# GpSimd's work on the weights tied to the steps of z, u's parts prepared a step earlier, and another order of the last pair

## What is computed

```python
theta = x @ w_theta
zr, zi = x * np.cos(theta), x * np.sin(theta)
y = einsum('ts,bsd->btd', w_tok_r, zr) + einsum('ts,bsd->btd', w_tok_i, zi)
u = x + y
u = u + np.maximum(u @ w_ch, 0.0)
h = np.maximum(u @ w_in, 0.0)
# conv over three neighbouring tokens, per channel, then
gate = 1.0 / (1.0 + np.exp(-conv_out))
out = (h * gate) @ w_out
```

## Time and profile before

| | us |
|---|---|
| median of 3 runs | 525.27 |
| lowest, highest | 524.72, 525.97 |
| the profiled execution, whole | 525.06 |
| its span, first to last instruction | 523.3 |
| TensorE busy (matmul) in the span | 507.9 |
| DVE, ACT, GpSimd busy | 441.4, 328.4, 89.7 |

### The profile page before, as it was taken

The page is one execution under the profiler, slowest core; times in us unless marked ns, Lnnn a source line. Parts: engine busy times, 40 slices in busy tenths (PEclk is TensorE's granted clock), DMA queues, the critical chain, the costliest instruction groups (busy, mean ns, idle before and its releaser), DMA issues.

```text
span 523.3 us, 10574 instructions
## 1 busy us (share of the span) xinstructions
PE 507.9 (97%) x4022; PEld 497.4 (95%) x4022; DVE 441.4 (84%) x682; ACT 328.4 (63%) x599; POOL 89.7 (17%) x76
## 2 busy tenths in 40 slices
PE   8999999999999998999799999999999999999997
PEld 7989898999999998999699999999999999999996
DVE  8999997999898869889588876898888888788783
ACT  4889887755534444354235364787777688678764
POOL 5988984000000142012000000000000000000000
PEclk9999999999999999999989999999999999999999
DMA  8999997999420732025600568002411002001102
GB/s 327 340 323 313 342 317 182 286 326 225 149 91 1 223 135 95 1 104 139 240 3 1 188 271 321 34 2 98 174 45 47 2 0 91 0 1 46 46 1 90
DMA packets 38114, 73.54 MB, mean 141 GB/s; under 512 B 6448, under 2 KB 23856, under 8 KB 38064
## 3 DMA queue, kind: packets, MB, share of 16 engines
q1 hardware_dynamic: 37344, 71.69, 41.2%
q10 hardware_dynamic: 720, 1.18, 0.6%
HBM read 52.80 MB, written 20.05 MB: 139 GB/s over the span
## 4 chain that ended last, share of the span: by engine, by line
PE 81%; DVE 9%; ACT 4%; DMA 3%; issue 2%; SPq 1%; POOL 0%; DVEq 0%; ACTq 0%
PE y_bank L1811 22%; PE y_bank L1897 17%; PE x_bank L1883 9%; PE theta_bank L1883 7%; PE y_bank L1842 7%; PE x_bank L1798 6%; PE weighed L1718 4%; PE x_sum L1676 4%; PE x_sum L1691 2%; DMA u_scratch<-u_part 2%; PE turned L1703 2%; DVE u_part L1502 1%; PE turned L1723 1%; PE x_sum L1662 1%; DVE angle L1432 1%
## 5 line engine op out<-in xcount | busy, mean ns | idle before, releaser
L1811 PE MATMUL y_bank<-rest_w,z 128*128 128x384 f32 x432 | 76.8, 335 | 1.5 <-DVE z L1460 1.5
L1811 PE MATMUL y_bank<-first_w,z 128*128 128x384 f32 x432 | 76.9, 334 | 0.3 <-issue 0.3
L1811 PEld LDWEIGHTS y_bank<-rest_w,z 128*128 128x128 f32 x432 | 74.9, 188 | 2.2 <-DVE z L1460 2.1
L1811 PEld LDWEIGHTS y_bank<-first_w,z 128*128 128x128 f32 x432 | 75.0, 188 | 0.5 <-issue 0.5
L1842 PE MATMUL y_bank<-u_part,channel_w 128*128 128x384 f32 x216 | 42.2, 345 | 4.2 <-DVE u_part L1502 4.2
L1137 ACT ACTIVATE sine<-angle 128x384 f32<-128x384 f32 x24 | 12.6, 526 | 52.3 <-DVE angle L1435 52.3
L1842 PEld LDWEIGHTS y_bank<-u_part,channel_w 128*128 128x128 f32 x216 | 39.1, 195 | 5.1 <-DVE u_part L1502 5.1
L1798 PE MATMUL x_bank<-theta_w,x_t 128*128 128x384 f32 x216 | 41.5, 335 | 0.2 <-DVE x_t L1417 0.2
L1798 PEld LDWEIGHTS x_bank<-theta_w,x_t 128*128 128x128 f32 x216 | 37.7, 188 | 0.7 <-DVE x_t L1417 0.7
L1718 PE MATMUL weighed<-q_scaled,k_scaled 64*128 64x128 f32 x384 | 31.6, 283 | 1.4 <-POOL q_scaled L986 1.0
L1718 PEld LDWEIGHTS weighed<-q_scaled,k_scaled 64*128 64x128 f32 x384 | 28.4, 187 | 4.1 <-issue 2.5
(11 more groups left out here) (213 smaller groups left out, 1215.9 us busy)
## 6 DMA issues: line engine op xcount, KB each, us to landing
u_scratch<-u_part SPq DMA_DIRECT2D x12, 768.0 KB, 4.3
first_w<-u_scratch SPq DMA_DIRECT2D x8, 768.0 KB, 7.7
a_in<-in_a_rows SPq DMA_DIRECT2D x15, 390.0 KB, 6.1
k_in<-in_k_rows SPq DMA_DIRECT2D x15, 384.0 KB, 6.0
q_in<-in_q_rows SPq DMA_DIRECT2D x14, 384.0 KB, 5.4
v_in<-in_v_tokens SPq DMA_DIRECT2D x16, 288.0 KB, 4.9
x_blocks<-x_scratch SPq DMA_DIRECT2D x12, 288.0 KB, 6.8
y<-x_even SPq DMA_DIRECT2D x6, 576.0 KB, 3.0
```

The lines of the kernel that those rows point to most:

```text
L1811: ins = pe.matmul(y_bank[2 * d + half][:, 0:HALF], z[s % 2][part][zp][:, d * P:(d + 1) * P], mixing_w(part, wp, s)[:, half_tokens(half)], ...
```

## The change

Three things are changed, all of them in order and waiting:

- **GpSimd's work on the weights** moves from `spare` to a `prepare_u` of its own, at spot 1 of steps 0 to 4, and starts in each with a wait for the split of z of the next tile, `z_low.done(pool, (b + 1) * T + s + 1)` (the b there is one less than the batch that is mixed). The two operations of double width are cut in two, so there are nine subtractions and four sums, 13 operations of 128 x 512. Tables `W_ROUNDED`, `W_SPLIT` and `W_COMBINED` say where each lies, by (batch mixed, step). The last two parts now belong to batch 3, and SP's load of w_out, which overwrites them, moves from step 0 to step 2 of batch 3, ahead of `load_u(0)`.
- **u's parts** are rounded, split, combined and stored from step 0 on: ACT's parts 0 and 1 stand at spot 0 of step 0 (before: spot 1 of step 0), the last at spot 0 of step 3 (before: step 4); DVE's splits and subtractions lie one or two spots to a step and a half earlier, the last at spot 1 of step 3; SP stores at spot 1 of steps 1 and 3 (before: 2 and 4). ACT waits for just as many subtractions as a part needs.
- **The last pair** of the feed-forward part: ACT rounds the odd tile's g ahead of the sigmoid of the even tile. DVE applies the odd tile's gate ahead of conv3 of the even tile, and splits the odd g ahead of the even tile's gate product.

```diff
@@ mix_batch @@
-            if b and not last:
+            if b:
                 do.spare(b, s)
@@ tables @@
-    N_W, N_U = 7, 5
+    N_W, N_U = 9, 5
-    W_OF = {(1, 2): (0,), (1, 3): (1,), (1, 4): (2,), (2, 2): (3, 4), (2, 3): (5, 6)}
+    W_PARTS = ("a12", "a22", "a11", "s1", "s3", "s2", "s4", "even", "odd")
+    W_ROUNDED = {(1, 1): (0, 1), (1, 3): (2,), (2, 1): (3,), (2, 2): (4, 5), (2, 3): (6,), (3, 0): (7, 8)}
+    W_SPLIT = {(1, 2): (0,), (1, 3): (1,), (1, 4): (2,), (2, 2): (3,), (2, 3): (4,), (2, 4): (5, 6), (3, 1): (7,), (3, 2): (8,)}
+    COMBINED = ("s1", "s3", "s2", "s4")
+    W_COMBINED = {(1, 4): (0,), (2, 0): (1,), (2, 1): (2,), (2, 2): (3,)}
@@ SP @@
-            if (s, spot) == (2, 1):
+            if (s, spot) == (1, 1):
                 u_split.done(sp, b, 3)
...
-            if (s, spot) == (4, 1):
+            if (s, spot) == (3, 1):
                 u_split.done(sp, b)
...
         def prepare(s):
-            if s == 0:
+            if s == 2:
                 sp.wait_ge(w_low, N_W)
                 sp.dma_start(out_rows[:, :, :], w_out.rearrange("(a p) n -> p a n", p=P)).then_inc(out_w_got, 16)
                 sp.dma_start(taps[:, :, :], taps_in).then_inc(taps_got, 16)
-            if s == 2:
                 mixed.done(sp, LAST * T + 1)
                 load_u(0)
@@ GpSimd @@
+        def split_w(m):
+            part = W_PARTS[m]
+            high, low = ff_w[part]
+            pool.wait_ge(w_high, m + 1)
+            pool.tensor_tensor(low, W_RAW[part], high.bitcast(F32), ALU.subtract).then_inc(w_low, 1)
+
+        def combine_w(i):
...
+            pool.wait_ge(w_low, 3)
+            if i:
+                pool.wait_ge(w_added, i)
+            pool.tensor_tensor(out, left, right, op).then_inc(w_added, 1)
+
+        def prepare_u(b, s, spot):
+            if spot == 1 and s < T - 1:
+                z_low.done(pool, (b + 1) * T + s + 1)
+                for m in W_SPLIT.get((b + 1, s), ()):
+                    split_w(m)
+                for i in W_COMBINED.get((b + 1, s), ()):
+                    combine_w(i)
@@ ACT @@
+            if m >= 3:
+                u_combined.done(act, b, 2 * m - 4)
             if m == 3:
-                u_combined.done(act, b)
...
-            for m in {(0, 1): (0, 1), (1, 1): (2,), (3, 1): (3,), (4, 0): (4,)}.get((s, spot), ()):
+            for m in {(0, 0): (0, 1), (0, 1): (2,), (2, 1): (3,), (3, 0): (4,)}.get((s, spot), ()):
                 round_u(b, m)
@@ ACT, step @@
+            if m == FF_STEPS - 1:
+                round_g(m, 1)
             if shapes:
                 gate(m, 0)
...
-            if shapes:
+            if m < FF_STEPS - 1:
                 round_g(m, 1)
@@ DVE @@
-            for m in {(1, 0): (0,), (1, 1): (1,), (2, 0): (2,), (4, 0): (3,), (4, 1): (4,)}.get((s, spot), ()):
+            for i in {(1, 1): (0, 1), (2, 0): (2,), (2, 1): (3,)}.get((s, spot), ()):
+                combine(b, i)
+            for m in {(0, 1): (0, 1), (1, 0): (2,), (3, 0): (3,), (3, 1): (4,)}.get((s, spot), ()):
                 split_part(b, m)
-            for i in {(2, 1): (0,), (3, 0): (1,), (3, 1): (2, 3)}.get((s, spot), ()):
-                combine(b, i)
@@ DVE, step @@
                 conv2(m, 0)
+            if m == FF_STEPS - 1:
+                apply_gate(m, 1)
+            if shapes:
                 conv3(m, 0)
+            if m == FF_STEPS - 1:
+                split_g(m, 1)
...
-            if shapes:
+            if m < FF_STEPS - 1:
                 apply_gate(m, 1)
...
             if shapes:
                 apply_gate(m, 0)
+            if m < FF_STEPS - 1:
                 split_g(m, 1)
```

More of the change, by code:

```diff
@@ L752, in layer @@
     U_COUNT = [16 * (4 + 1 + b % 2) for b in range(LAST)]
[L754 to L765 removed]
+    W_RAW = {"a12": w_raw[:, 1, :, 0, :], "a22": w_raw[:, 1, :, 1, :], "a11": w_raw[:, 0, :, 0, :], "s1": w_raw[:, 1, :, 1, :],
+             "s3": w_raw[:, 0, :, 1, :], "s2": w_raw[:, 0, :, 0, :], "s4": w_raw[:, 1, :, 0, :],
+             "even": w_raw[:, 2, :, 0, :], "odd": w_raw[:, 2, :, 1, :]}
+    W_PARTS = ("a12", "a22", "a11", "s1", "s3", "s2", "s4", "even", "odd")
[3 more added lines that the diff above has]
+    W_COMBINED = {(1, 4): (0,), (2, 0): (1,), (2, 1): (2,), (2, 2): (3,)}
     block = ctx.enter_context(nc.Block())
@@ L1013, in select @@
                                pattern=[[0, len(BLOCKS_OF) - EARLY], [1, CHUNK]], channel_multiplier=-1).then_inc(selected.sem, 1)
-        def spare(b, s):
-            for m in W_OF.get((b, s), ()):
-                pool.wait_ge(w_high, m + 1)
-                raw, (high, low) = w_part_of(m)
-                pool.tensor_tensor(low, raw, high.bitcast(F32), ALU.subtract).then_inc(w_low, 1)
-            a11, a21, a12, a22 = (w_raw[:, d, :, m, :] for d in range(2) for m in range(2))
-            if (b, s) == (2, 0):
-                pool.wait_ge(w_low, 3)
-                pool.tensor_tensor(a22, a21, a22, ALU.add).then_inc(w_added, 1)
-                pool.tensor_tensor(a21, a11, a21, ALU.subtract).then_inc(w_added, 1)
-            if (b, s) == (2, 1):
-                pool.wait_ge(w_added, 2)
-                pool.tensor_tensor(a11, a22, a11, ALU.subtract).then_inc(w_added, 1)
-                pool.wait_ge(w_added, 3)
-                pool.tensor_tensor(a12, a12, a11, ALU.subtract).then_inc(w_added, 1)
+        def split_w(m):
[4 more added lines that the diff above has]
+        def combine_w(i):
+            a11, a21, a12, a22 = (w_raw[:, d, :, m, :] for d in range(2) for m in range(2))
+            out, left, right, op = ((a22, a21, a22, ALU.add), (a21, a11, a21, ALU.subtract), (a11, a22, a11, ALU.subtract),
+                                    (a12, a12, a11, ALU.subtract))[i]
+            pool.wait_ge(w_low, 3)
[9 more added lines that the diff above has]
+                    combine_w(i)
         def pad(n):
@@ L1053, in _ @@
         pool.memset(quarter[:, :], PI / 2).then_inc(const, 1)
-        program(pool, Work(scale_q=scale_q, scale_k=scale_k, select=select, spare=spare, begin=begin))
+        program(pool, Work(scale_q=scale_q, scale_k=scale_k, select=select, prepare_u=prepare_u, begin=begin))
     @block.scalar
@@ L1153, in spare @@
         def spare(b, s):
-            for m in W_OF.get((b, s), ()):
+            for m in W_ROUNDED.get((b, s), ()):
+                part = W_PARTS[m]
                 act.wait_ge(w_got, 16)
-                if m == 3:
-                    act.wait_ge(w_added, 4)
-                if m == 4:
+                if part in COMBINED:
+                    act.wait_ge(w_added, COMBINED.index(part) + 1)
+                if part == "s3":
                     all_stored_late(act, 0)
-                raw, (high, _) = w_part_of(m)
-                act.activation(high, raw, ACT.Copy).then_inc(w_high, 1)
+                act.activation(ff_w[part][0], W_RAW[part], ACT.Copy).then_inc(w_high, 1)
         def round_u(b, m):
```

9 lines of the change are left out of this document (removed).

## The result

The changed kernel takes 519.48 us (median of 4 runs, 518.84 to 520.63) where the kernel before takes 525.37 (4 runs, 524.72 to 525.97): ratio 0.9891, 95% interval 0.9869 to 0.9912, so 5.7 us faster by the ratio. The forecast was 517.8, in a range from 515.9 to 521.0. The profiled execution took 519.45 us (span 517.5), against 525.06 before. In the changed kernel the mixing product is at L1822, the channel product at L1853, the feed-forward product at L1894, the last pair's at L1908; z's split is at L1465, u's at L1529 and L1507, its sums at L1537.

What follows compares the result with a forecast made beforehand. TensorE, busy 507.9 of 523.3 us, was taken as the bound, leaving idle stretches, clock and ends to win. Terms -2.50 - 3.96 - 0.25 - 0.76 = -7.47 us gave 517.8 us, range 515.9 to 521.0.

Steps and rivals of the forecast that it cites:

- Part 3: Batch 3, last weights and SP's queue: later loads cost 0 with two us to spare; earlier out_w splits give -0.25 us.
- case (a): Whole kernel as summed: 517.8 us, 516.9 to 519.3 with batch 2's residual between 0.6 and 3; chance 0.60.
- case (c): Steps 0 to 4: DVE becomes the bound, stalls in two more batches; 520.8, up to 522.5 us; chance 0.13.
- signs named for a wrong forecast: A mixing product of batch 1 waits for z, or ACT waits for u_scratch near 310 us.
- Part 1: Steps 0 to 4: u's parts earlier take the sums' store off the path, costing nothing without GpSimd; cover 1.0 us at thinnest.
- the lock: DVE and GpSimd share an SBUF port pair, held for a whole instruction while the other side blocks.
- Part 2: GpSimd behind z's split: batch 1 gains 2.50 us; batch 2 gains 5.46 but pays 1.5 in held DVE operations, -3.96.
- case (b): Batch 2: GpSimd finds no way in, or only into DVE's idle time; 516.3 us; chance 0.18.
- rival (e): SP's queue at 200 GB/s lands 13.8 us late before the first feed-forward steps; slower, 531.6 us; chance 0.05.
- Below 340 GB/s: SP's queue in batch 3: rate under which moving its 6.7 MB (19.7 us) would cost something.
- Part 4: Last feed-forward pair: the odd tile's split comes 1.0 us earlier, removing TensorE's idle time, -0.76 us; even tile hidden.

Runs made afterwards that it cites:

- u_late: Changed kernel with u's roundings, splits, subtractions and stores back at their old steps; 518.14 us, ratio 0.9875 to the kernel before.
- no_pool_wait: Changed kernel without GpSimd's waits for the split of z; 517.95 us, ratio 0.9860 to the kernel before.
- pool_in_gaps: Changed kernel with GpSimd's four sums in batch 1 and four subtractions in batch 2 gathered behind z of step 5; 517.75 us, ratio 0.9863 to the kernel before.
- old_last_pair: Changed kernel with the old order of gate, rounding and split in the last feed-forward pair; 521.83 us, ratio 0.9925 to the kernel before.
- u_late_rest_mended: Changed kernel with u's work at its old steps, GpSimd's sums and subtractions gathered behind z, load_u(0) issued before SP's wait; 520.82 us, ratio 0.9928.
- after_again: The changed kernel unedited, run again on another chip beside its variants; 519.96 us, ratio 0.9901 to the kernel before.
- sums_first: Changed kernel with load_u(0) sent behind the store of the last sums on SP's queue; 521.13 us, ratio 0.9936 to the kernel before.

## Why the forecast came out as it did

**The point and the range.** 519.48 lies 1.7 us over the point and inside the range; the sum was -7.47, and -5.6 came. The two batches and the last pair give -6.95 against a forecast of -7.22; nearly all that is missing is Part 3, +1.7 against -0.25. The result lies 0.2 above the band of case (a), whose width was for batch 2. The range had room for it through case (c), which did not come; it was not laid for what happened, so that the result lies inside is in part luck. One of the signs named for a wrong forecast did come: ACT waited for u_scratch near 310 us (3.95 us idle, up to 312.5).

**What bounds the kernel.** Right: the lost time was in batch 1's end, in batch 2, its clock fall and the last pair. The estimate of a batch without a wait, 56.36, is met by batch 1 at 56.42, and the channel product of batch 2 took 9.63 us at a clock of 1.00, where it took 11.21 before.

**Part 1.** Right in size, half wrong in its cause. Batch 1 took 56.42 (forecast 56.36), and z's first half, prepared in steps 0 to 4, was there 1.3, 0.9, 1.6, 1.7 and 0.8 us before TensorE took it (158.9, 167.1, 174.3, 181.9, 189.1 against 160.25, 168.04, 175.84, 183.65, 189.9) where 1.4, 1.1, 1.7, 1.9 and 1.0 were forecast. In batch 3, with a GpSimd operation beside it, 0.6 were left in step 2 (289.7 against 290.33). The cover was thin, and held. But I let the store carry most of the stall, as the chain shows it in 4.81 of its microseconds. u_late, with the store and without the lock, loses only 0.8 us in batch 1. The largest row of a chain is not what its removal is worth; what runs beside it and ends a little earlier bounds that. no_pool_wait is the other side: with the store gone and the lock kept, 1.9 us are lost.

**Part 2.** Right, and case (a) against (b) was decided as put down: each of the GpSimd operations shown comes in after the first DVE operation. The strict reading of the order of issue, by which GpSimd would stay out until DVE's queue pauses, gives case (b), and that did not come. Forecast were 1.15 us at the first pair and 1.0 at the second; 1.1 and 1.0 came. TensorE's steps in batch 2 (7.80 when undisturbed) ran 0, 0.25, 0.28 and 0.12 us long, and the wait before the last was 0.45 us: 1.7 in all with what follows, forecast 1.5. The forecast had its largest wait, 0.8 us, before the last mixing, where 0.45 came. pool_in_gaps confirms the cause by taking 1.4 away. Case (c) did not come: no mixing product outside batch 2 waited for z.

**Part 3 is the step that failed**, in its size and its sign: +1.7 instead of -0.25. It is the mechanism of rival (e) in a small form, but not by the rate that I had made its condition: the queue moved 404 GB/s from 294 to 310 us, more than I took. Two terms were wrong. The first is when out_rows leaves, 292.05 and not 290. The rows of DVE, GpSimd and TensorE in steps 1 to 3 of batch 3 of the changed kernel:

```profile
282.01 2.12 DVE L1537 TENSOR_TENSOR u_sum<-u_sum 128x384 f32<-128x384 f32 x2
282.23 1.49 POOL L1014 TENSOR_TENSOR in_w<-out_rows,in_w 128x512 fp32r<-128x512 f32 x1 [31.38 <-DVE z L1465]
...
289.17 1.24 DVE L1465 TENSOR_TENSOR z<-z_full,z 128x384 fp32r<-128x384 f32 x2
...
290.48 1.54 POOL L1014 TENSOR_TENSOR in_w<-out_rows,in_w 128x512 fp32r<-128x512 f32 x1 [6.77 <-DVE z L1465]
...
290.33 6.40 PE L1822 MATMUL y_bank<-rest_w,z 128*128 128x384 f32 x36
```

z is whole at 290.41, 0.1 us after TensorE began on its first half; before, it was whole at 295.18 for a product that began at 296.76, 1.6 ahead. In batch 1 of the changed kernel, with u's early work and no GpSimd operation in the step before, the same z was whole 0.9 ahead (174.94 against 175.84). So u's work takes 0.7 of these 1.7 us; the other 1.0 is GpSimd's own operation at 282.23, which made the two subtractions last 2.12 instead of 1.14. Part 1 had worked out that u's work makes z later within its step, and Part 2 that a GpSimd operation does; Part 3 took z at its old place in the step. The second term is the transfer. From the issue to the first data pass some 2 us, and from the last data (about 310.6) to ACT's start another 1.9; I had divided bytes by rate alone. Sum: 292.05 + 2 + 16.6 + 1.9 = 312.5, which is when ACT started, against a need at 310.0 (forecast 309.7). Of these 2.5 us late, 1.96 reached TensorE. The store in the earlier trace rows already held some of what was left out: its 1.57 MB at 387 GB/s are 4.1 us, and it took 4.81. "Below 340 GB/s" was the wrong condition, and the two us to spare behind a sum of 17 did not cover what the sum left out.

**Part 4.** Right: the wait is gone in the changed kernel and back by 0.8 us in old_last_pair. The split of the odd tile runs from 506.95 us, and that of the even one is done at 510.7, when TensorE takes it at 511.2: 0.5 to spare, 0.7 forecast.

**What stays open.** The first profile of the changed kernel has a wait of 1.96 and that of pool_in_gaps one of 2.7 us without any fall of the clock, while in five profiles, that of before among them, it fell at waits of 2.2 to 3.4. What decides this wasn't tried. Nor was it tried why the first mixing of batch 1 starts between 150.8 and 152.7 us from one kernel to the next; it moves single profiles by a microsecond, whatever is changed behind it.

## What to carry to other kernels

When a change adds a wait, follow every queue behind the waiting instruction, cost a queued transfer from its issue to the start of its reader, and let what needs nothing of the wait go ahead of it (here 2 to 3 us for two moved lines), but only if it is ready by then: with u's stores a step later the same two lines cost time. In this kernel GpSimd's operations cost least where DVE waits for another engine; just behind the DVE operation that feeds TensorE they cost 1.4 us of batch 2. Carry the lateness that one part of a change causes into the sum of the next, and try its halves apart, since each can take the other's cover away.

## What the runs showed of the hardware

A GpSimd operation that becomes ready while one DVE operation runs gets in before DVE's next, though DVE's queue has no pause: in the rows shown of batches 2 and 3, with 1.0 to 1.1 us more for a pair, and 0.5 more for a single operation of 0.36 us. L1428 under the same GpSimd operation was not held (0.55 us for 0.52).

6.7 MB on SP's queue moved at 404 GB/s and still took 20.5 us from the first issue to the reader. A store of 1.57 MB took 13.54 us behind 5.1 MB, 5.8 when it was issued 6.5 us later, and 4.8 with nothing ahead.

At one wait of TensorE of 2.2 to 3.4 us, in stages where it is otherwise always busy, the granted clock fell for some microseconds, to 0.50 at its lowest (1.2 GHz), in five of the profiled executions: after the wait in before, old_last_pair, u_late_rest_mended and after_again, during its last 1.5 us in sums_first. It cost 1.6 us in after_again and as much in before (11.21 us for a channel product of 9.56); after 2.7 us in another execution the clock stayed at 2.4 GHz.
